# Experts as native float32 matmuls from an eight-slot weight ring, and a GpSimd that splits both matrices of the MLP

## What is computed

```python
# attention: batch 4, 8 heads, 576 positions, head size 64 -> x [2304, 512]
scores = q @ k.T / 8                      # masked: local (32 back) or strided (every 32nd)
x = softmax(scores) @ v

# experts: D = 512, E = 8, F = 1024
do_compute = x @ w_skip > 0               # the other tokens pass unchanged
xc = x[do_compute]
logits = xc @ w_gate
e_idx, gate_w = argmax(logits), softmax(logits)[argmax]
for e in range(E):
    h = maximum(xc[e_idx == e] @ w1[e], 0)
    y[e_idx == e] = gate_w * (h @ w2[e])
out = x.copy(); out[do_compute] = xc + y

# MLP on all 2304 tokens: 512 -> 2048 -> 512
h = out @ w_in
result = maximum(0.01 * h, h) @ w_out
```

## Time and profile before

| | |
|---|---|
| median of 3 runs | 816.52 us (816.3 to 817.72) |
| span of the profiled execution | 812.8 us |
| PE busy | 725.0 us, 89% of the span |
| DVE busy | 416.4 us, 51% |
| ACT busy | 346.3 us, 43% |
| POOL busy | 125.9 us, 15% |
| moved by DMA | 91.09 MB, mean 112 GB/s |

### The profile page before, as it was taken

How to read it: one execution, slowest core, us unless ns; L and a number is a source line. 1 busy time by engine, 2 the same in 40 slices (tenths; PEclk the granted TensorE clock), 3 DMA queues, 4 the chain that set the end, 5 groups by cost and what they waited for, 6 DMA issues and landing times.

```text
span 812.8 us, 13496 instructions
## 1 busy us (share of the span) xinstructions
PE 725.0 (89%) x4627; PEld 669.0 (82%) x4627; DVE 416.4 (51%) x781; ACT 346.3 (43%) x669; POOL 125.9 (15%) x114
## 2 busy tenths in 40 slices
PE   3989989963687799996699999999999999999997
PEld 2888889853687799995599998999999999999996
DVE  4766748664888888886332234223333332333222
ACT  4688776431454477775122232222322222223222
POOL 2120134024624511110300100100100010000000
PEclk9999979895898899998699999999999999999999
DMA  8584664793566678886300120120011012001001
GB/s 176 120 180 104 157 173 120 244 358 112 198 220 218 199 232 266 253 259 226 116 1 1 40 78 0 40 79 1 10 50 58 0 39 77 0 0 40 1 0 40
DMA packets 75165, 91.09 MB, mean 112 GB/s; under 512 B 25809, under 2 KB 46801, under 8 KB 75122
## 3 DMA queue, kind: packets, MB, share of 16 engines
q1 hardware_dynamic: 70386, 78.66, 32.8%
q0 software_dynamic: 3680, 11.86, 4.7%
q10 hardware_dynamic: 1056, 0.02, 0.1%
HBM read 73.88 MB, written 16.65 MB: 111 GB/s over the span
## 4 chain that ended last, share of the span: by engine, by line
PE 73%; SPq 9%; DVE 6%; issue 5%; DMA 4%; ACT 3%; POOL 0%; ACTq 0%; DVEq 0%; POOLq 0%
PE psum L1605 25%; PE psum L1622 24%; PE psum L1531 6%; SPq L415 5%; PE psum L1517 5%; PE psum L1533 2%; SPq L410 2%; DVE hp L1225 2%; PE psum L1519 2%; DMA x_rows<-xo 2%; PE psum L1455 1%; PE psum L1472 1%; SPq L400 1%; PE psum L1542 1%; PE psum L1357 1%
## 5 line engine op out<-in xcount | busy, mean ns | idle before, releaser
L1295 DVE SCALAR_TENSOR_TENSOR g_act<-g_raw 128x384 f32<-128x384 f32 x96 | 53.7, 559 | 221.1 <-ACT g_raw L964 220.6
L964 ACT ACTIVATE g_raw<-psum 128x384 f32<-128x384 f32 x96 | 47.2, 492 | 236.8 <-PE psum L1605 236.8
L1605 PE MATMUL psum<-x2h,wih 128*128 128x384 f32 x384 | 131.6, 343 | 1.4 <-DVE x2l L1277 1.4
L1605 PE MATMUL psum<-x2h,wil 128*128 128x384 f32 x384 | 130.2, 339 | 0.0
L1605 PE MATMUL psum<-x2l,wih 128*128 128x384 f32 x384 | 129.7, 338 | 0.0
L1622 PE MATMUL psum<-wh,g_l 128*128 128x512 f32 x288 | 114.0, 396 | 0.0
L1622 PE MATMUL psum<-wl,g_h 128*128 128x512 f32 x288 | 113.7, 395 | 0.0
L1622 PE MATMUL psum<-wh,g_h 128*128 128x512 f32 x288 | 112.2, 389 | 0.5 <-DVE g_l L1299 0.5
L1186 DVE TENSOR_TENSOR wl<-raw,wh 128x1024 fp32r<-128x1024 f32 x67 | 90.9, 1359 | 13.6 <-ACT wh L861 13.2
L1531 PE MATMUL psum<-hp,wh 128*128 128x320 f32 x256 | 78.6, 376 | 20.9 <-DVE hp L1225 20.7
L1299 DVE TENSOR_TENSOR g_l<-g_act,g_h 128x384 fp32r<-128x384 f32 x96 | 53.7, 559 | 57.0 <-ACT g_h L971 57.0
(11 more groups left out here) (163 smaller groups left out, 1177.7 us busy)
## 6 DMA issues: line engine op xcount, KB each, us to landing
raw<-in_moe_w_dram SPq DMA_DIRECT2D x64, 512.0 KB, 4.0
q_st<-in_q_dram SPq DMA_DIRECT2D x8, 576.0 KB
k_st<-in_k_dram SPq DMA_DIRECT2D x8, 576.0 KB
x<-x_rows SPq DMA_DIRECT2D x6, 768.0 KB, 5.4
y_rows<-zrow SPq DMA_DIRECT2D x1, 4480.0 KB
x_sb<-x_rows SPq DMA_DIRECT2D x4, 1024.0 KB, 6.2
wi_raw<-in_moe_w_in_dram POOLq DMA_DIRECT2D x4, 1024.0 KB, 5.8
raw<-in_moe_w_out_dram SPq DMA_DIRECT2D x8, 512.0 KB, 3.8
```

The lines of the kernel that those rows point to most:

```text
L964: act.activation(g_raw[:, f % 2, :], bank[f % 2][:, 0:MT * P], ACT.Copy).then_inc(s_mr, 1)
L1295: dve.scalar_tensor_tensor(out=g_act[:, f % 2, :], in0=g_raw[:, f % 2, :], scalar=LEAK, in1=g_raw[:, f % 2, :], op0=ALU.mult, op1=ALU.max) ...
L1605: last = pe.matmul(bank[f % 2][:, 0:MT * P], wt[:, c, f * P:(f + 1) * P], xp[:, T.par, c, :], start=(c == 0 and n == 0), stop=(c == KD - 1 ...
```

## The change

- The parts `wh`, `wl` of the expert weights and the ring `raw` of four slots go. In their place stands `wring`, eight slots of 128x1024 float32: a whole expert. SyncE refills a slot as soon as the matmuls that read it are done (`half_done`), in the order 0, 2, 1, 4, 3, 6, 5, 7, and waits for the zero filling of `y_rows` before the first refill.
- `hidden` and `share` use the float32 weights and float32 activations directly: one native matmul of 160 columns for each block in place of a pair.
- ScalarE does the relu straight from PSUM into `hp`; `hb`, `ht` and both splits are gone. The gathered tokens and the output are copied once, one half on ScalarE and one on VectorE.
- GpSimd splits nothing during attention. During the eight tiles it loads and splits `w_in` (four pieces) and then `w_out` (four pieces) through a `stage` of two slots of 1 MB, the next piece being loaded while one is split. SyncE no longer loads `w_out`. The parts of `w_out` are now `woh` and `wol`.
- Buffers of the MLP lie at other addresses. The instructions of attention, routing and MLP are the same otherwise.

The core of the diff:

```diff
     def half_load(eng, e_, n):
-            u_, to = n // 2, raw[:, n % 4, :]
+            u_, to = n // 2, wring[:, n, :]
...
-            eng.dma_start(to, src).then_inc(s_raw[n % 4], 16)
+            eng.dma_start(to, src).then_inc(s_w[n], 16)
# sync
             for n in range(4, 2 * NU):
-                sp.wait_ge(s_wl, n - 3)
                 half_load(sp, 0, n)
...
-                def slot_free(n):
-                    k_ = i0 * 2 * NU + ((d + 1) * 2 * NU + n - 3)
-                    sp.wait_ge(s_wh, k_)
-                    sp.wait_ge(s_wl, k_)
+                def half_done(n):
+                    k_ = i0 * FC + (d * FC + 2 * (n // 2) + 2)
+                    sp.wait_ge(s_l2 if n % 2 else s_l1, k_)
...
-                    for n in range(2 * NU):
-                        y_before(n)
-                        slot_free(n)
+                    for n in (0, 2, 1, 4, 3, 6, 5, 7):
+                        if n == 1:
+                            y_before()
+                        half_done(n)
                         half_load(sp, ex_, n)
                 with sp.Else():
-                    for n in range(2 * NU):
-                        y_before(n)
-                        slot_free(n)
-                        sp.dma_start(raw[:, n % 4, :].rearrange("p (c n) -> p c n", n=D),
-                                     w_out_c[:, 2 * n:2 * n + 2, :]).then_inc(s_raw[n % 4], 16)
+                    y_before()
+            sp.wait_ge(s_zd, 32)
# gpsimd
-            for n in range(5):
-                pool.wait_ge(s_raw[n % 4], 16 * (n // 4 + 1))
-                split(half(wh, n), half(wl, n), raw[:, n % 4, :], s_wh, s_wl, n + 1)
...
+            stage_load(0)
+            for i in range(2 * NU):
                 pool.wait_ge(s_xt, 2 * (i + 1))
                 gather_x(i + 1)
-                pool.wait_ge(s_wi, 16 * (i + 1))
-                w_ = slice(i * (F2 // NU), (i + 1) * (F2 // NU))
-                split(wih[:, :, w_], wil[:, :, w_],
-                      wi_raw[:, :].rearrange("p (c f) -> p c f", f=F2 // NU), s_wih, s_wil, i + 1)
-                pool.wait_ge(s_wil, i + 1)
+                if i + 1 < 2 * NU:
+                    if i:
+                        pool.wait_ge(s_stl, i)
+                    stage_load(i + 1)
+                stage_split(i)
# scalar, in tile
-                    act.activation(hb[:, f % 2, :], bank[f % 2][:, TILE:2 * TILE], ACT.Copy
-                                   ).then_inc(s_hb, 1)
+                    if not (first and f < 4):
+                        act.wait_ge(s_l2, T.n(FC, f - 3))
+                    act.activation(hp[:, f % 4, :], bank[f % 2][:, 0:TILE], ACT.Relu
+                                   ).then_inc(s_hp, 1)
...
-                for c in (0, 2):
-                    act.activation(yb[:, c:c + 2, :], Y[:, c:c + 2, TILE:2 * TILE], ACT.Copy
-                                   ).then_inc(s_ya, 1)
+                if not first:
+                    act.wait_ge(s_yt, T.n(2, 0))
+                act.activation(yt[:, 0:2, :], Y[:, 0:2, 0:TILE], ACT.Copy).then_inc(s_ya, 1)
# vector, in tile: ht, half_lo, relu's low part and the two adds go
+                if not first:
+                    y_rows(T.i0 + (T.d - 1))
+                x_copy(T.i0 + (T.d + 1), 1 - par)
+                dve.wait_ge(s_l2, T.n(FC, FC))
+                if not first:
+                    dve.wait_ge(s_yt, T.n(2, 0))
+                dve.tensor_copy(yt[:, 2:4, :], Y[:, 2:4, 0:TILE]).then_inc(s_yv, 1)
# tensor, hidden
-                    pe.matmul(bank[f % 2][:, 0:2 * TILE], wh[:, u_, w_], xt[:, T.par, c, :],
-                              start=(c == 0), stop=False)
-                    last = pe.matmul(bank[f % 2][:, 0:TILE], wl[:, u_, w_], xt[:, T.par, c, 0:TILE],
-                                     start=False, stop=(c == KD - 1))
+                    last = pe.matmul(bank[f % 2][:, 0:TILE], wring[:, 2 * u_, w_], xt[:, T.par, c, :],
+                                     start=(c == 0), stop=(c == KD - 1))
# tensor, share
-                    pe.matmul(Y[:, c, 0:2 * TILE], wh[:, u_, w_], hp[:, f % 4, :],
-                              start=(f == 0), stop=False)
-                    last = pe.matmul(Y[:, c, 0:TILE], wl[:, u_, w_], hp[:, f % 4, 0:TILE],
-                                     start=False, stop=(f == FC - 1))
+                    last = pe.matmul(Y[:, c, 0:TILE], wring[:, 2 * u_ + 1, w_], hp[:, f % 4, :],
+                                     start=(f == 0), stop=(f == FC - 1))
```

More of the change, by code:

```diff
@@ L118, in attention_experts_mlp @@
     zrow = at(keep, "zrow", [FILL, D])
-    wh = at(keep, "wh", [P, NU, 2048], F32R)
-    wl = at(keep, "wl", [P, NU, 2048], F32R)
-    raw = at(keep, "raw", [P, 4, 1024])
+    ring0 = keep[0]
+    wring = at(keep, "wring", [P, 2 * NU, 1024])
     region_a = keep[0]
@@ L193, in attention_experts_mlp @@
     e = [a2[0]]
-    wi_raw = at(e, "wi_raw", [P, 2048])
+    stage = at(e, "stage", [P, 2, 2048])
     xg = at(e, "xg", [HALF, 2, D])
[L196 to L200, removed]
+    xt = at(e, "xt", [P, 2, KD, TILE])
+    hp = at(e, "hp", [P, 4, TILE])
     yt = at(e, "yt", [P, KD, TILE])
@@ L267, in attention_experts_mlp @@
         s_plan = sem("s_plan")
[L269 to L274, removed]
+        s_w = [sem(f"s_w{i}") for i in range(2 * NU)]
+        s_st = [sem("s_st0"), sem("s_st1")]
+        s_sth = sem("s_sth")
+        s_stl = sem("s_stl")
         s_tick = sem("s_tick")
@@ L855, in _, with x_copy @@
                                ).then_inc(s_hot, 1)
[L858 to L871, removed]
+            def x_copy(j, par):
+                act.wait_ge(s_xt, 2 * j + 1)
+                act.activation(xt[:, par, :, 0:HALF],
+                               bank[2][:, 0:KD * HALF].rearrange("d (c t) -> d c t", c=KD),
+                               ACT.Copy).then_inc(s_xf[0], 1)
             act.wait_ge(s_plan, 2)
@@ L940, in _ @@
             y_rows(last_tile)
-            for n in (5, 6, 7):
-                half_hi(n, tiles * 32 + 32)
             def x2_hi(m, j, par):
@@ L966, in mstep @@
                     act.wait_ge(s_mg, T.n(FC2, f + 1))
-                    if T.first and f == 0:
-                        act.wait_ge(s_wl, tiles * 8 + 8)
                     if not (T.first and f < 2):
@@ L1209, in tile @@
                 first, par = T.first, T.par
-                for f in range(FC):
-                    dve.wait_ge(s_hb, T.n(FC, f + 1))
-                    if not (first and f < 2):
-                        dve.wait_ge(s_hl, T.n(FC, f - 1))
-                    dve.tensor_tensor(ht[:, f % 2, :], bank[f % 2][:, 0:TILE], hb[:, f % 2, :],
-                                      ALU.add).then_inc(s_ht, 1)
-                    if f == 4:
-                        x_lo(T.i0 + (T.d + 1), 1 - par)
-                    if f == 1 and not first:
-                        y_rows(T.i0 + (T.d - 1))
-                    def weights(n=5 + f):
-                        half_lo(n % (2 * NU), T.n(8, n + 1))
-                    def relu(f=f):
-                        dve.wait_ge(s_hh, T.n(FC, f + 1))
-                        dve.scalar_tensor_tensor(out=hp[:, f % 4, TILE:2 * TILE], in0=ht[:, f % 2, :],
-                                                 scalar=0.0, in1=hp[:, f % 4, 0:TILE].bitcast(F32),
-                                                 op0=ALU.max, op1=ALU.subtract).then_inc(s_hl, 1)
-                    for stage in ((weights, relu) if f < FC - 1 else (relu, weights)):
-                        stage()
-                for c in (0, 2):
-                    dve.wait_ge(s_ya, T.n(2, c // 2 + 1))
-                    if not first and c == 0:
-                        dve.wait_ge(s_yt, T.n(2, 0))
-                    dve.tensor_tensor(yt[:, c:c + 2, :], Y[:, c:c + 2, 0:TILE], yb[:, c:c + 2, :],
-                                      ALU.add).then_inc(s_yv, 1)
+                if not first:
+                    y_rows(T.i0 + (T.d - 1))
+                x_copy(T.i0 + (T.d + 1), 1 - par)
+                dve.wait_ge(s_l2, T.n(FC, FC))
+                if not first:
+                    dve.wait_ge(s_yt, T.n(2, 0))
+                dve.tensor_copy(yt[:, 2:4, :], Y[:, 2:4, 0:TILE]).then_inc(s_yv, 1)
             tile(Tile(0, 0))
@@ L1257, in _ @@
             y_rows(last_tile)
-            for n in (5, 6, 7):
-                half_lo(n, tiles * 8 + n + 1)
             def x2_rows(m):
@@ L1613, in mshare @@
                 if T.first and f == 0:
-                    pe.wait_ge(s_wl, tiles * 8 + 8)
+                    pe.wait_ge(s_stl, 2 * NU)
                 if f == 0 and not T.first:
```

122 lines of the change are left out of this document (56 added, 66 removed).

## The result

The changed kernel takes 782.43 us (median of 4 runs, 782.1 to 783.94), the kernel before 816.41 us (4 runs beside it, 813.73 to 817.72). The ratio is 0.96, with a 95% interval of 0.9576 to 0.9624. The change is worth 34 us; the forecast was 23, and the lower end of its range, 786, lies 3.6 us above the time measured. The sign was right, the size was not.

A forecast was written before the change was run, and what follows sets the result against it. GpSimd's subtraction holding VectorE was taken to slow the early expert tiles. Experts falling from 177.5 to 156.2 us save 21.3, start 1.5, end 0.5: 23.3 off a span of 812.8, plus 3.7, gives 793 us; range 786 to 802.

The forecast's parts named there:

- What bounded the kernel: Early expert tiles: five waits for VectorE held by GpSimd's subtraction, 20.7 us, plus slow-clock stretches, 9.3 us, of 32 lost.
- The native matmul: Experts: 0.137 us per record of 160 columns, 0.274 us per block, 17.5 us per tile, replacing pairs of 0.257 us.
- the line through the earlier trace: Attention's native matmuls: 0.110 us a record at 126 columns, 0.065 at 72, extended to 160 columns.
- at 0.110 a record: Rival, experts: native matmul cheaper, tile of 15.9 us until DMA sets 18.8; 788 us, chance 0.05.
- at 0.343 a block: Rival, experts: four passes cost as columns do, tile of 23.8 us; 828 us, chance 0.03.
- The tile: Experts: 17.5 us of matmuls, 1.76 of transposes and 0.1 of remainder make 19.4 us per tile.
- The end: After the experts' last matmul: output copies side by side, 1.0 us less, but unexplained pause kept; gain 0.5 us.
- Start: First tile's tokens: no refills beside their second half, and one copy for two parts; gain 0.4 to 2.5, taken 1.5 us.
- From span to time: Whole kernel: runs lie 3.7 us above the span, so a span of 789.5 us becomes 793.2.
- MLP, GpSimd, SyncE, DMA: MLP length unchanged; GpSimd busy about 12 of 19.4 us per tile; refills in time; DMA shortfall taken as 0.
- The rival of DMA setting the pace: Experts: 304 GB/s asked against 287 to 313 seen, costing up to 8 us; 801 us, chance 0.09.

The follow-up runs named there:

- b_nosplit: Kernel before, GpSimd's cast and subtraction of w_in during the experts left out, wih loaded by DMA, wil not made: 788.25 us against 815.17, ratio 0.9677.
- a_dve_relu: Kernel after, ScalarE copying each hidden block to SBUF and VectorE computing the relu with two SBUF operands: 806.33 us, ratio 0.9887.
- a_lastloads: Kernel after, with SyncE refilling the eight weight slots in the last tile too (weights read by nobody): 789.23 us, ratio 0.9682.
- a_dve_sbuf1: Kernel after, ScalarE copying each hidden block to SBUF and VectorE computing the relu from one SBUF operand: 794.97 us, ratio 0.9731.

## What the prediction made of it, point by point

The mechanism held. What failed is the sum: three of its terms had the wrong size, the length of a tile, the pause at the end of the experts, and the step from span to time.

**What bounded the kernel: right, with two slips in the reading.** Five waits and the slow clock were named as 30 of 32 lost us. Taking away GpSimd's work alone gave 27 us (b_nosplit), and putting a held instruction into the native kernel cost 24 (a_dve_relu). Both directions are shown. But "Each is followed by a stretch at clock 0.50" is true of four of the five only: behind the second, of 1.25 us, the clock stayed at 1.00, and the five lengths in that sum are these four and the start. And I put all five down to a relu's low part held by the subtraction, which is so for three; one was held by the cast, and one stood behind a held `wl`. The change takes away all of them, so the forecast did not suffer.

**The native matmul: right.** From 277.23 to 278.32, in PE's timeline of the kernel after, eight records take 1.09 us:

```profile
276.36 1.04 PE L1455 MATMUL psum<-ident,yt 128*80 128x128 f32 x8
277.23 1.25 PE L1431 MATMUL psum<-xt,wring 128*128 128x160 f32 x8
278.32 1.25 PE L1445 MATMUL psum<-hp,wring 128*128 128x160 f32 x8
...
281.58 0.72 PE L1414 MATMUL psum<-ident,xg 80*128 80x80 f32 x8
282.13 1.29 PE L1431 MATMUL psum<-xt,wring 128*128 128x160 f32 x8
```

That is 0.136 us a record against 0.137 from the line through the earlier trace rows; the rivals at 0.110 a record and at 0.343 a block fall. (The latter's bound, "slower than before from 0.315 us per block on", should read 0.32: 23.3 us over 512 blocks is 0.046 more than 0.274.)

**The tile: too long, because of its small terms.** "with the transposes, 0.72 + 1.04 us, a tile should take 18.2, and takes 18.3: the model holds to 0.1 us" is the step that failed. The transposes are given by their durations there, while the matmuls are given from start to start. A group's duration takes in the drain of its last member, beside which the next group already runs. In the rows above the groups follow each other after 0.55 us (282.13 - 281.58) and 0.87 us (277.23 - 276.36), 1.42 together, not 1.76. A tile is 64 x 0.272 + 1.42 = 18.8 us; measured 18.85. With 19.4 I was 0.55 too high per tile, 4.4 us in eight; 1.0 of it was given back, mostly by the slow first stretch, which costs 2.7 to 2.9 us instead of 2.0 (the first 24 records take 5.97 us from start to start; at 0.136 each they would take 3.3). The fit with the kernel before was chance: 16.42 + 1.42 = 17.84 against 18.3 leaves 0.46 us per tile. Most of it is small waits of `share` for `hp`: two of its blocks in each of these tiles start 0.22 to 0.31 us after the record ahead of them instead of 0.07, each time just after `hp` was ready, and the records beside them are some 0.04 us apart more than usual. They hid in my 0.34 of drain and 0.1 of remainder, and I carried them into a kernel that has no such wait. 3.4 of the 10.6 us of error.

**The end: "so the gain is 0 to 1, I take 0.5": wrong, 4.0.** The mechanism that I had named, the shorter chain of the output, gave its 0.8. I had taken the pause behind it for a fixed price because the trace gives no releaser. It fell from 4.57 to 1.6 us (start to start). Loads put back into the last tile of the native kernel bring 2.0 us of it back (a_lastloads), but cutting them in the kernel before took away no more than b_nosplit lost without touching them, so the reason stays open in part. The transposes behind the shorter pause took 0.8 instead of 1.5 us from start to start, at a clock of 1.00 where it had been 0.50. A stall without a releaser has unknown bounds, not zero: the upper end of the range should have held all of its 4.3 us. 3.5 us of error.

**Start: right in its mechanism, 2.1 us for 1.5.** The second half of the tokens came 1.37 us behind the first instead of 3.37, with no refills beside it; no run tests whether they were the reason.

**From span to time: "Runs lie 3.7 us above the span": wrong.** An execution of the kernel before takes 1.8 us more than its span: 814.59 us for a span of 812.8, 815.17 for 813.4, 817.75 for 816.0. I had compared the span of an execution from the short end with the median of others. After, the difference is 2.2 us; the profiled execution took 783.94 for 781.7, and it was the longest of its four, so that the median lies only 0.7 above the span. About 3 us of error: a comparison of a span with a median mixes two executions, which differ by some us.

**MLP, GpSimd, SyncE, DMA: right.** 0.3 us for 0; nothing waits for GpSimd, which is busy for 9.3 us per tile (46.92 in five), less than the 12 said; the refills were never late. The rival of DMA setting the pace was given 0.09 on a ceiling that isn't one.

The errors are 3.4 (experts) + 3.5 (end) + 0.6 (start) + 0.3 (MLP) + 3.0 (span to time) = 10.8 us, which is 793.2 - 782.4; from the 793 that the forecast was rounded to, 10.6. All five have the same sign. The range was made as if they were independent: its low side held the matmul's cost and DMA's floor, but neither the transposes' overlap nor the pause.

## What to carry to other kernels

A small VectorE instruction that reads float32 from SBUF in the critical chain of a kernel is a hazard as soon as GpSimd does long elementwise work beside it, and each of GpSimd's instructions can hold one; let it read PSUM, or give it to ScalarE. Build a model of a pipelined engine from starts alone, and where it is checked against a stage, look for small waits that it would count as work. Take the offset between span and time from one and the same execution, and give a pause without a releaser a range from nothing to all of it.

## What the runs showed of the hardware that I had not expected

- GpSimd's float32 subtraction also holds a VectorE instruction with a single SBUF operand (244 ns alone, up to 4566 held), and held none with its operand in PSUM (323 to 327 ns in 64).
- GpSimd's cast (1.9 us, one operand) holds VectorE as the subtraction does: 2.65 us for an instruction of 0.33 (a_dve_relu), 2.01 for one of 0.32 (the kernel before).
- At 160 moving columns a native float32 product (0.272 us per block) costs 6% more than three products in the split form (0.257 us). A stage with the splitting work left out took 151.5 us split and 151.8 native.
- The profile's DMA share passed 1 (1.14 at 361 GB/s) with no sign of a limit for TensorE.
- The pause of PE at the end of the native kernel's loop grew from 1.6 to 3.6 us when loads of 512 KB ran beside it.
- Behind eight pauses of 1.2 to 1.6 us in a dense stage the granted clock stayed at 1.00 (a_dve_sbuf1). Of six pauses of about 2.4 to 2.5 us (a_dve_relu) four had a stretch of 3.2 to 3.6 us at 0.5 behind them, and two had none.
